# The earliest best cluster by halving sums on GpSimd, in place of a second maximum on VectorE

## The chip, the cores and the metric

The kernel runs on one core of one Trainium2 chip. The metric is the device time of one execution in microseconds (us). Engines are named as in the profile: PE is TensorE (PEld its weight loads), DVE is VectorE, ACT is ScalarE, POOL is GpSimd, SP is SyncE, which here issues all transfers.

## The reference

Clustered attention, then two feed-forward blocks, all in float32. Two batches, 8 heads, 768 positions, head dimension 64, 16 clusters. Each query and each key is assigned to the cluster whose centroid it is most similar to; a query attends only to keys of its own cluster. Where two clusters are equally good, `argmax` gives the earlier one.

```python
q_assign = np.argmax(np.einsum('bhsd,hcd->bhsc', q_n, c_n), axis=-1)
k_assign = np.argmax(np.einsum('bhsd,hcd->bhsc', k_n, c_n), axis=-1)
mask = q_assign[:, :, :, None] == k_assign[:, :, None, :]
scores = np.where(mask, 0.125 * np.matmul(q, k.transpose(0, 1, 3, 2)), -1e9)
attn = softmax(scores) @ v                     # 2 x 8 x 768 x 64
x = attn as 1536 x 512
x = ((x @ w1) * (x @ w2)) @ w3 @ w_out         # 1024 wide inside
h = x @ w_in                                   # 2048 wide
out = (np.maximum(h, 0) + alpha * np.minimum(h, 0)) @ w_out2
```

## The kernel before

Each engine has its own program, written out by hand; semaphores join them. Every product is made from high and low halves of its operands, in three matmuls or, for the scores, four.

**Stages.** A setup (about 70 us) loads and splits weights, multiplies the two middle matrices into one, and prepares the first heads. Attention follows, to about 295 us, then the feed-forward blocks.

**Attention.** The 16 heads are taken in 4 turns of 4 heads; a head has 6 tiles of 128 queries, so a turn has 24 tiles, and `step(it, c, last)` is one tile's step on each engine: each engine has its own version, and the order inside it is the engine's queue. PE in step c makes the scores of tile c (`score`), transposes probabilities of group c - 4 (`turn_probabilities`, line 689, in two halves b = 0, 1), does what `prepared` lists, and multiplies group c - 5 with v (`weigh`). DVE in step c takes the row maximum of tile c (`maximum`, line 1200), then the low halves `pl` of group c - 4 (`probabilities_lo`, line 1206, a pair of instructions), then what `prepared` lists, then in one step of six the reciprocal of the row sums (`inverse`, line 1212). ACT makes exponentials, the high halves `ph`, and copies of finished output (line 982). PE's transposition of group g, half b, waits for `pl` of group g - 1, half b. POOL handles clusters (`picks`), the split of v (lines 489, 493), the addition of epsilon to the row sums (line 531), and adds, scales and splits the finished output of two heads (lines 541, 545, 551, 558).

**Clusters.** Once in 12 steps, for two heads together. PE makes the similarities (steps 2 and 3 of 12), DVE transposes them so that each of 128 partitions holds 24 positions with 32 values (`ct`, line 1181). Then, before the change:

1. POOL adds the high and low contributions: 24 x 16 values `c16` (line 509, step 4).
2. DVE takes their maximum over 16, `cmx` (line 1190, step 4).
3. POOL subtracts it, compares with zero, and multiplies by the weights 16, 15, ..., 1 (lines 511, 513, 514). A best cluster keeps its weight, the others are 0.
4. DVE takes a second maximum (line 1193, step 6): the weight of the earliest best one.
5. POOL adjusts it (518), subtracts it (519) and turns the result into the rows `oh` by maximum and multiplication (521): query rows and key rows get values such that their product in the scores pushes pairs of different clusters far down.
6. DVE transposes `oh` back (line 1196, step 8), and SP sends eight small transfers of it into the operands of the two heads (`masks`, line 327). PE waits for them at the first tile of each head.

Between some POOL instructions stands a small one of 1 x 2 elements into `spare` (lines 512, 517, 520). POOL waits for each of its own instructions by a semaphore before it starts the next of the chain (`ordered_step`).

The places of this work in a turn are given by `prepared`, which all engines use: "pick1" in step 4 of 12, "pick2" in step 6, "pick3" in step 8.

Of the kernel before, what the change touches and what calls it, by code (L numbers as in the profile page):

```python
# [34 lines left out]
FAR = 2.0 ** 60  # L35
SCALE = D ** -0.5
HB = 4
# [10 lines left out]
FILLS = 6  # L48
# [6 lines left out]
def prepared(it, c, last):  # L55

    j, m = c // 12 * 2, c % 12
    plan = {0: [("turned", j + 3, 0)], 1: [("turned", j + 3, 1)], 2: [("cluster", j + 2, 0)], 3: [("cluster", j + 2, 1)],
            4: [("pick1", j + 2, 0)], 6: [("pick2", j + 2, 0)], 8: [("pick3", j + 2, 0)],
            10: [("turned", j + 4, 0)], 11: [("turned", j + 4, 1)]}.get(m, [])  # L60
    there = HB if last else 2 * HB if isinstance(it, int) and it == TURNS - 2 else 3 * HB
    return [(kind, head, half) for kind, head, half in plan if head < there]
# [7 lines left out]
def finished(c):  # L70

    j, u = divmod(c - T6 - LX, T6)
    return (j, u) if 0 <= j < HB else (None, None)
# [8 lines left out]
def inverted_now(c, last, lag):  # L82

    j, t = divmod(c - T6, T6)
    return j if t == lag and j >= 0 and (not last or j < HB) else None


def build(nc, q, k, v, cen, w1, w2, w3, wo, w_in, w_out, alpha, out):
    ctx = ExitStack()
    with ctx:  # L90
        def sem(name):
            return ctx.enter_context(nc.semaphore(name))

        def sb(name, shape, dt=F32, where=ctx):
            return where.enter_context(nc.sbuf_tensor(name, shape, dt))
# [17 lines left out]
        zero = al[:, NJ:NJ + T6]  # L113
# [116 lines left out]

        block = ctx.enter_context(nc.Block())

        POOL_SETUP = 16 + HB
        CEN_DVE = 6
        CLUS = 9
        W12_EARLY = len(W12_STEPS)
        W34_EARLY = NF + 1
        X_FREE, FOLD_FREE = 2, 1
# [209 lines left out]
        def _(pool):  # L448
            count = [0]

            def ordered(ins):
                count[0] += 1
                ins.then_inc(setup_pool, 1)
                pool.wait_ge(setup_pool, count[0])
# [3 lines left out]
                                            base=0, pattern=[[-1, P]], channel_multiplier=1))  # L458
# [2 lines left out]
            ordered(nc.gpsimd.memset(scl[0:D, :], SCALE))  # L461
            ordered(nc.gpsimd.memset(zero[:, :], 0.0))
            ordered(nc.gpsimd.memset(epsilon[:, :], 1e-9))
            ordered(nc.gpsimd.iota(wts[:, :], pattern=[[-1, NCL]], base=NCL, channel_multiplier=0,
                                   allow_small_or_imprecise_dtypes=True))
            for j in range(1, HB):
                ordered(nc.gpsimd.memset(cwin[j][:, :].bitcast(F32), 0.0))
            ordered(nc.gpsimd.memset(oh[:, :, :, :], 0.0))
            ordered(nc.gpsimd.memset(far[:, 0:1], 0.0))
            ordered(nc.gpsimd.memset(far[:, 1:3], 1.0))  # L470
            for e in range(2):
                ordered(nc.gpsimd.memset(far[64 * e:64 * e + 32, 0:1], -1.0))
                ordered(nc.gpsimd.memset(far[64 * e:64 * e + 32, 1:2], FAR))
                ordered(nc.gpsimd.memset(far[64 * e:64 * e + 32, 2:3], 0.0))
            assert count[0] == POOL_SETUP

            def window(it, j):
# [16 lines left out]
                                        v12[e][:, :, x_rows(j)].bitcast(F32), ALU.subtract).then_inc(v_done, 1)  # L494
                pool.wait_ge(v_done, n + 1)

            def picks(it, j, part):

                pair = 2 * it + j // 2
                ct3 = ct[:, :].rearrange("p (b c) -> p b c", c=32)  # L500
                over = lambda x: x[:, :].unsqueeze(2).to_broadcast([P, 24, NCL])
                weights = wts[:, :].unsqueeze(1).to_broadcast([P, 24, NCL])
                def ordered_step(k, ins):
                    ins.then_inc(clus_step, 1)
                    pool.wait_ge(clus_step, CLUS * pair + k)

                if part == 1:
                    pool.wait_ge(prep_free, FILLS * (pair + 1))
                    ordered_step(1, nc.gpsimd.tensor_tensor(c16[:, :, :], ct3[:, :, 0:NCL], ct3[:, :, NCL:2 * NCL], ALU.add))
                    pool.wait_ge(clus_step, CLUS * pair + 2)  # L510
                    ordered_step(3, nc.gpsimd.tensor_tensor(c16[:, :, :], c16[:, :, :], over(cmx), ALU.subtract))
                    nc.gpsimd.tensor_tensor(spare[0:1, 0:2], zero[0:1, 0:2], zero[0:1, 0:2], ALU.add)
                    ordered_step(4, nc.gpsimd.tensor_scalar(c16[:, :, :], c16[:, :, :], 0.0, None, ALU.is_ge))
                    ordered_step(5, nc.gpsimd.tensor_tensor(c16[:, :, :], c16[:, :, :], weights, ALU.mult))
                else:
                    pool.wait_ge(clus_step, CLUS * pair + 6)
                    nc.gpsimd.tensor_tensor(spare[0:1, 0:2], zero[0:1, 0:2], zero[0:1, 0:2], ALU.add)
                    ordered_step(7, nc.gpsimd.tensor_scalar(cmx[:, :], cmx[:, :], far[:, 2:3], None, ALU.subtract))
                    ordered_step(8, nc.gpsimd.tensor_tensor(c16[:, :, :], c16[:, :, :], over(cmx), ALU.subtract))
                    nc.gpsimd.tensor_tensor(spare[0:1, 0:2], zero[0:1, 0:2], zero[0:1, 0:2], ALU.add)  # L520
# [42 lines left out]
            def step(it, c, last):  # L563
                j, t = divmod(c, T6)
                out_head, u = finished(c)
                for kind, h, _ in prepared(it, c, last):
                    if kind in ("pick1", "pick2"):
                        picks(it, h, int(kind[4]))
# [26 lines left out]
            picks(0, 0, 1)  # L595
            picks(0, 0, 2)
            split_v(0, 0)
            for c in range(LEAD):
                step(0, c, False)
# [522 lines left out]
        def _(dve):  # L1122
# [61 lines left out]
            def picks(it, j, part):  # L1184


                pair = 2 * it + j // 2
                if part == 1:
                    dve.wait_ge(clus_step, CLUS * pair + 1)
                    nc.vector.tensor_reduce(cmx[:, :], c16[:, :, :], AX.X, ALU.max).then_inc(clus_step, 1)  # L1190
                elif part == 2:
                    dve.wait_ge(clus_step, CLUS * pair + 5)
                    nc.vector.tensor_reduce(cmx[:, :], c16[:, :, :], AX.X, ALU.max).then_inc(clus_step, 1)
                else:
                    dve.wait_ge(clus_step, CLUS * pair + CLUS)
                    nc.vector.transpose(ct[:, 0:HS], oh[:, 0, :, :].rearrange("p b c -> p (b c)")).then_inc(onehot_done, 1)
# [52 lines left out]
            picks(0, 0, 2)  # L1249
            picks(0, 0, 3)  # L1250
            w3_lo_part(6, 0)
            for half in range(2):
# [108 lines left out]
```

## Time and profile before

| what | value |
|---|---|
| median of 3 runs | 747.94 us (747.90 to 747.99) |
| the profiled execution | 747.64 us, its span 745.8 us |
| PE busy | 739.0 us (99%), granted clock 0.999 |
| DVE, ACT, POOL busy | 411.8, 311.6, 179.5 us |
| SP | issues all transfers; the 16 DMA engines moved 54 MB |
| chain that ended last | PE 97%, DVE 1%, DMA 1% |

The span runs from the first instruction to the last; the time has another 1.8 us around it. A start time is counted from the span's start. Durations overlap a little: an instruction can start before the one ahead of it on its engine has fully ended, so that start to start is shorter than the sum of durations. Lines of the profile with "x2" or "x6" hold that many instructions of one kind in a row.

### The profile page before, as it was taken

Reading aid. Unit: us, or ns where it says so; the run is one execution under the profiler, and the core shown is the slowest. Engines: PE = TensorE matmul, PEld = TensorE weight load, DVE = VectorE, ACT = ScalarE, POOL = GpSimd, SP = SyncE. Lnnn points to the kernel's source line nnn. Section 1 sums busy time; section 2 is a strip of 40 time slices with the busy share of each in tenths; the row PEclk is TensorE's granted clock in tenths of the full one; section 3 lists DMA queues with packets and bytes.
Section 4 is the critical chain, followed back from the end, with each engine's and each line's share of the span. In section 5 each row is a group of like instructions: output and inputs, shape, how many; then the busy total and the mean of one; then the engine's idle time right before and its main releaser. Section 6 shows DMA issues by size and latency. Waiting matters only on the chain.

```text
span 745.8 us, 10690 instructions
## 1 busy us (share of the span) xinstructions
PE 739.0 (99%) x3792; PEld 641.6 (86%) x3792; DVE 411.8 (55%) x632; ACT 311.6 (42%) x623; POOL 179.5 (24%) x211
## 2 busy tenths in 40 slices
PE   8999999999999999999999999999999999999998
PEld 6888999999999998888888888888888888888886
DVE  4435999999999984721311432575434333343432
ACT  5235988988988884311211422432012111121111
POOL 2141566866865893500000000000000000000000
PEclk9999999999999999999999999999999999999999
DMA  9636366566566233300000022140001000010001
GB/s 293 195 94 144 78 152 155 124 146 154 127 146 153 65 84 92 98 29 1 1 0 1 20 93 85 57 130 11 1 0 57 1 0 1 1 56 1 1 0 57
DMA packets 65371, 54.17 MB, mean 73 GB/s; under 512 B 32032, under 2 KB 54576, under 8 KB 65328
## 3 DMA queue, kind: packets, MB, share of 16 engines
q1 hardware_dynamic: 65328, 53.59, 27.9%
q8 instruction: 28, 0.46, 0.3%
q14 instruction: 15, 0.12, 0.1%
HBM read 31.50 MB, written 3.19 MB: 47 GB/s over the span
## 4 chain that ended last, share of the span: by engine, by line
PE 97%; DVE 1%; DMA 1%; ACT 1%; issue 0%; SPq 0%; DVEq 0%; ACTq 0%
PE slot L625 63%; PE acc L625 24%; PE slot L689 9%; PE acc L638 1%; PE slot L737 1%; DMA early<-in_moe_w_out 1%; DVE xl L1163 0%; DVE xl L1145 0%; ACT xh L938 0%; ACT xh L945 0%; DVE abx L1283 0%; DVE ab L1279 0%; ACT abx L1055 0%; ACT asb L1041 0%; ACT ost L1108 0%
## 5 line engine op out<-in xcount | busy, mean ns | idle before, releaser
L625 PE MATMUL slot<-xh,w 128*128 128x512 f32 x768 | 248.0, 389 | 0.0
L625 PEld LDWEIGHTS slot<-xh,w 128*128 128x128 f32 x768 | 144.1, 188 | 29.8
L625 PE MATMUL slot<-xl,w 128*128 128x512 f32 x384 | 149.4, 389 | 0.0
L1101 ACT CAST gh<-gf 128x512 fp32r<-128x512 f32 x48 | 29.9, 623 | 203.2 <-PE acc L625 186.0
L1206 DVE TENSOR_TENSOR pl<-slot,ph 128x384 fp32r<-128x384 f32 x192 | 97.6, 549 | 8.5 <-ACT ph L973 8.2
L1200 DVE TENSOR_REDUCE nm<-slot 128x1 f32<-128x768 f32 x96 | 91.4, 952 | 15.4 <-PE slot L625 13.8
L973 ACT CAST ph<-slot 128x384 fp32r<-128x384 f32 x192 | 83.5, 489 | 34.3 <-PE slot L689 33.8
L965 ACT ACTIVATE pf<-slot,nm 128x768 f32<-128x768 f32 x96 | 88.4, 921 | 4.6 <-DVE nm L1200 4.5
L625 PEld LDWEIGHTS slot<-xl,w 128*128 128x128 f32 x384 | 72.1, 188 | 15.0
L625 PE MATMUL slot<-k,q 80*128 80x384 f32 (+1 forms) x384 | 82.9, 337 | 0.0
L1329 DVE TENSOR_TENSOR gl<-gf,gh 128x512 fp32r<-128x512 f32 x48 | 33.2, 692 | 89.9 <-ACT gh L1101 89.9
L689 PE MATMUL slot<-ident,pf 128*128 128x128 f32 x576 | 79.4, 273 | 0.2
L689 PEld LDWEIGHTS slot<-ident,pf 128*128 128x128 f32 x576 | 68.5, 140 | 5.4 <-DVE pl L1206 1.4
L625 PE MATMUL acc<-ph,v 128*128 128x384 f32 x192 | 71.7, 373 | 0.0
L625 PEld LDWEIGHTS slot<-k,q 80*128 80x128 f32 (+1 forms) x384 | 68.6, 188 | 0.3
L1279 DVE TENSOR_TENSOR ab<-slot,asb 128x512 f32<-128x512 f32 x24 | 16.5, 690 | 90.2 <-ACT asb L1041 90.2
L1322 DVE TENSOR_SCALAR neg<-slot,al 128x512 f32<-128x512 f32 x48 | 36.0, 750 | 52.1 <-PE slot L625 52.1
L625 PE MATMUL acc<-pl,v 128*128 128x384 f32 x192 | 64.7, 337 | 0.0
L625 PE MATMUL slot<-w,gh 128*128 128x512 f32 x192 | 59.1, 389 | 0.0
L625 PE MATMUL acc<-w,gh 128*128 128x512 f32 x192 | 59.1, 389 | 0.0
L1041 ACT COPY asb<-slot 128x512 f32<-128x512 f32 x24 | 14.1, 588 | 103.1 <-PE slot L625 103.1
L625 PEld LDWEIGHTS acc<-w,gh 128*128 128x128 f32 x192 | 36.0, 188 | 7.4
(121 smaller groups left out, 1012.0 us busy)
## 6 DMA issues: line engine op xcount, KB each, us to landing
stage<-in_moe_w SPq DMA_DIRECT2D x16, 256.0 KB, 3.5
stage<-in_moe_w_in SPq DMA_DIRECT2D x16, 256.0 KB, 2.7
stage<-in_moe_w_out SPq DMA_DIRECT2D x16, 256.0 KB, 3.0
stage<-in_moe_w SPq DMA_DIRECT2D x6, 512.0 KB, 4.2
qk<-in_q SPq DMA_DIRECT2D x16, 192.0 KB, 3.9
qk<-in_k SPq DMA_DIRECT2D x16, 192.0 KB, 3.9
vn<-in_v SPq DMA_DIRECT2D x16, 192.0 KB, 3.8
q<-k SPq DMA_DIRECT2D x16, 192.0 KB, 3.8
```

The lines of the kernel that those rows point to most:

```text
L625: return nc.tensor.matmul(o, a, b, start=start, stop=stop)
L638: last = nc.tensor.transpose(o[:, t * P:(t + 1) * P], qk[j % 2][:, 3 * half + t, :, :].rearrange("p a d -> p (a d)"), ident[:, :])
L689: last = nc.tensor.transpose(turned_p[:, b, i * P:(i + 1) * P], p[:, key_tile * P:(key_tile + 1) * P], ident[:, :])
L965: nc.scalar.activation(pf[c % NPF][:, :, :], wide(scores[c % 2]), ACT.Exp, bias=nm[:, c % 4:c % 4 + 1], accum_out=sm[j % 2][:, t:t + 1]).t ...
L973: copy(ph[g % NPH][:, b, :], turned_p[:, b, 0:HS]).then_inc(ph_done, 1)
L1041: copy(asb[f % 2][:, :], bank[2 * (f % 2)]).then_inc(asb_done, 1)
L1101: copy(gh[j % 2][:, :], gf[j % 2][:, :]).then_inc(gh_done, 1)
L1200: nc.vector.tensor_reduce(nm[:, c % 4:c % 4 + 1], wide(scores[c % 2]), AX.XY, ALU.max, negate=True).then_inc(max_done, 1)
L1206: tt_(pl[g % NPH][:, b, :], turned_p[:, b, 0:HS], f32(ph[g % NPH][:, b, :]), ALU.subtract).then_inc(pl_done, 1)
L1279: tt_(ab[f % 2][:, :], bank[2 * (f % 2) + 1], asb[f % 2][:, :], ALU.mult).then_inc(ab_done, 1)
L1322: ts(neg[:, :], h, 0.0, al[:, j:j + 1], ALU.min, ALU.mult).then_inc(neg_done, 1)
L1329: tt_(gl[j % 2][:, :], gf[j % 2][:, :], f32(gh[j % 2][:, :]), ALU.subtract).then_inc(gl_done, 1)
```

## The change

The weights 16 to 1 become powers of two, FAR times 2^16 down to FAR times 2 (FAR is 2^60). After the comparison and the multiplication, POOL adds up the 16 values of a position in four halvings (16 to 8, 4, 2, 1, written into unused columns of `oh`). In a sum of different powers of two the largest is more than half of the sum, so half of the sum separates the earliest best cluster from all others: POOL halves the sum, subtracts it, and makes `oh` by maximum and minimum. DVE's second maximum is gone, and with it step "pick2"; POOL does the whole of `picks` in step 4. DVE's transposition stays in step 8. Sixteen memsets make the weights in the setup where one `iota` did, and the constants `far` lose a column.

```diff
-            4: [("pick1", j + 2, 0)], 6: [("pick2", j + 2, 0)], 8: [("pick3", j + 2, 0)],
+            4: [("pick1", j + 2, 0)], 8: [("pick3", j + 2, 0)],
...
-            ordered(nc.gpsimd.iota(wts[:, :], pattern=[[-1, NCL]], base=NCL, channel_multiplier=0,
-                                   allow_small_or_imprecise_dtypes=True))
+            for c in range(NCL):
+                ordered(nc.gpsimd.memset(wts[:, c:c + 1], FAR * 2.0 ** (NCL - c)))
...
-            def picks(it, j, part):
+            def picks(it, j):
...
+                spot = oh[:, 1, :, :].rearrange("p b c -> p (b c)")
+                sums = [spot[:, 24 * n:48 * n].rearrange("p (b c) -> p b c", c=n) for n in (8, 4, 2, 1)]
+                total = sums[3].rearrange("p b c -> p (b c)")
...
                 ordered_step(5, nc.gpsimd.tensor_tensor(c16[:, :, :], c16[:, :, :], weights, ALU.mult))
-                else:
-                    pool.wait_ge(clus_step, CLUS * pair + 6)
-                    nc.gpsimd.tensor_tensor(spare[0:1, 0:2], zero[0:1, 0:2], zero[0:1, 0:2], ALU.add)
-                    ordered_step(7, nc.gpsimd.tensor_scalar(cmx[:, :], cmx[:, :], far[:, 2:3], None, ALU.subtract))
-                    ordered_step(8, nc.gpsimd.tensor_tensor(c16[:, :, :], c16[:, :, :], over(cmx), ALU.subtract))
-                    nc.gpsimd.tensor_tensor(spare[0:1, 0:2], zero[0:1, 0:2], zero[0:1, 0:2], ALU.add)
-                    ordered_step(9, nc.gpsimd.tensor_scalar(
-                        oh[:, 0, :, :].rearrange("p b (a c) -> p a b c", a=2),
-                        c16[:, :, :].rearrange("p (a b) c -> p a b c", a=2), far[:, 0:1], far[:, 1:2], ALU.max, ALU.mult))
+                k = 5
+                for n, (x, y) in enumerate(zip([c16] + sums, sums)):
+                    w = y.shape[2]
+                    ordered_step(k + n + 1, nc.gpsimd.tensor_tensor(y[:, :, :], x[:, :, 0:w], x[:, :, w:2 * w], ALU.add))
+                nc.gpsimd.tensor_tensor(spare[0:1, 0:2], zero[0:1, 0:2], zero[0:1, 0:2], ALU.add)
+                ordered_step(k + 5, nc.gpsimd.tensor_scalar(total, total, 0.5, None, ALU.mult))
+                ordered_step(k + 6, nc.gpsimd.tensor_tensor(c16[:, :, :], c16[:, :, :], over(total), ALU.subtract))
+                nc.gpsimd.tensor_tensor(spare[0:1, 0:2], zero[0:1, 0:2], zero[0:1, 0:2], ALU.add)
+                ordered_step(k + 7, nc.gpsimd.tensor_scalar(
+                    oh[:, 0, :, :].rearrange("p b (a c) -> p a b c", a=2),
+                    c16[:, :, :].rearrange("p (a b) c -> p a b c", a=2), far[:, 0:1], far[:, 1:2], ALU.max, ALU.min))
...
-                elif part == 2:
-                    dve.wait_ge(clus_step, CLUS * pair + 5)
-                    nc.vector.tensor_reduce(cmx[:, :], c16[:, :, :], AX.X, ALU.max).then_inc(clus_step, 1)
```

## Rows read from the trace of the kernel before

**Rows 1.** Busy times by window: stretch, PE, PEld, DVE, ACT, POOL, clock, DMA.

```profile
120.00:160.00 40.00, 40.00 (x271) 38.99 (x270) 38.50 (x68) 33.93 (x80) 24.98 (x33) 1.00 0.67 152
```

**Rows 2.** Timeline of DVE: start us, duration us, engine, line, operation.

```profile
129.37 0.96 DVE L1200 TENSOR_REDUCE nm<-slot 128x1 f32<-128x768 f32 x1
...
131.18 0.54 DVE L1193 TENSOR_REDUCE cmx<-c 128x24 f32<-128x384 f32 x1
131.64 0.95 DVE L1200 TENSOR_REDUCE nm<-slot 128x1 f32<-128x768 f32 x1
...
135.33 0.57 DVE L1196 STREAM_TRANSPOSE ct<-oh 128x384 f32<-128x384 f32 x1
...
136.66 1.00 DVE L1206 TENSOR_TENSOR pl<-slot,ph 128x384 fp32r<-128x384 f32 x2
...
138.66 1.01 DVE L1206 TENSOR_TENSOR pl<-slot,ph 128x384 fp32r<-128x384 f32 x2
```

**Rows 3.** Timeline of PE and its weight loads, same pair of heads.

```profile
131.80 0.42 PE L625 MATMUL acc<-ph,v 128*128 128x384 f32 x1
...
134.03 0.19 PEld L625 LDWEIGHTS acc<-ph,v 128*128 128x128 f32 x1 [0.16 <-ACT xf L982]
...
138.24 0.49 PE L638 MATMUL acc<-ident,qk 128*128 128x128 f32 x3
...
140.62 0.49 PE L638 MATMUL acc<-ident,qk 128*128 128x128 f32 x3
...
141.64 0.86 PE L625 MATMUL slot<-k,q 128*128 128x384 f32 x4
```

**Rows 4.** Timeline around 71 us, where PE waited for DVE.

```profile
70.60 1.02 DVE L1206 TENSOR_TENSOR pl<-slot,ph 128x384 fp32r<-128x384 f32 x2
...
71.68 0.31 PEld L689 LDWEIGHTS slot<-ident,pf 128*128 128x128 f32 x3 [0.15 <-DVE pl L1206]
...
71.98 0.42 PE L625 MATMUL acc<-ph,v 128*128 128x384 f32 x1
```

**Rows 5.** Line 509 by itself: ns min/median/max, first and last start.

```profile
L509 POOL TENSOR_TENSOR c<-ct x8: 1008/1014/1022, 35.1 to 236.2; 128x384 f32<-128x384 f32 x8
```

**Rows 6.** Timeline of POOL, the pair of rows 2 and 3.

```profile
129.86 1.02 POOL L514 TENSOR_TENSOR c<-c,wts 128x384 f32<-128x384 f32 x1
131.80 0.18 POOL L517 TENSOR_TENSOR spare<-al 1x2 f32<-1x2 f32 x1 [0.92 <-DVE cmx L1193]
...
133.48 1.64 POOL L521 TENSOR_SCALAR oh<-c,far 128x384 f32<-128x384 f32 x1
```

**Rows 7.** Groups of POOL: shapes, count, busy us, mean ns, idle before.

```profile
L545 POOL TENSOR_TENSOR xf<-xf,rep 128x768 f32<-128x768 f32 x8 | 18.8, 2350 | 0.6
...
L513 POOL TENSOR_SCALAR c<-c 128x384 f32<-128x384 f32 x8 | 9.4, 1172 | 0.0
...
L558 POOL TENSOR_TENSOR xl<-xf,xh 128x768 f32 x4 | 7.4, 1838 | 0.7 <-POOL xh L551 0.7
```

**Rows 8.** Timelines of POOL and DVE in the setup.

```profile
42.39 0.18 POOL L517 TENSOR_TENSOR spare<-al 1x2 f32<-1x2 f32 x1 [2.09 <-DVE cmx L1193]
...
44.08 1.64 POOL L521 TENSOR_SCALAR oh<-c,far 128x384 f32<-128x384 f32 x1
...
45.75 0.58 DVE L1196 STREAM_TRANSPOSE ct<-oh 128x384 f32<-128x384 f32 x1 [3.51 <-POOL oh L521]
```

**Rows 9.** Timelines of POOL and DVE at the first place in attention.

```profile
76.31 0.18 POOL L517 TENSOR_TENSOR spare<-al 1x2 f32<-1x2 f32 x1 [0.73 <-DVE cmx L1193]
...
77.99 1.64 POOL L521 TENSOR_SCALAR oh<-c,far 128x384 f32<-128x384 f32 x1
...
79.81 0.57 DVE L1196 STREAM_TRANSPOSE ct<-oh 128x384 f32<-128x384 f32 x1
```

**Rows 10.** DMA issues: size, us to landing; and the fourth mask transfer on SP.

```profile
q<-ct SPq DMA_DIRECT2D x4, 24.0 KB, 1.9
...
137.84 0.59 SPq L327 DMA_DIRECT2D k<-ct  x1
```

More of the change, by code:

```diff
@@ L231, in build @@
         block = ctx.enter_context(nc.Block())
-        POOL_SETUP = 16 + HB
+        POOL_SETUP = 13 + NCL + HB
         CEN_DVE = 6
-        CLUS = 9
+        CLUS = 12
         W12_EARLY = len(W12_STEPS)
@@ L469, in _ @@
             ordered(nc.gpsimd.memset(far[:, 0:1], 0.0))
-            ordered(nc.gpsimd.memset(far[:, 1:3], 1.0))
+            ordered(nc.gpsimd.memset(far[:, 1:2], FAR))
             for e in range(2):
                 ordered(nc.gpsimd.memset(far[64 * e:64 * e + 32, 0:1], -1.0))
-                ordered(nc.gpsimd.memset(far[64 * e:64 * e + 32, 1:2], FAR))
-                ordered(nc.gpsimd.memset(far[64 * e:64 * e + 32, 2:3], 0.0))
+                ordered(nc.gpsimd.memset(far[64 * e:64 * e + 32, 1:2], 0.0))
             assert count[0] == POOL_SETUP
@@ L495, in split_v @@
                 pool.wait_ge(v_done, n + 1)
-            def picks(it, j, part):
+            def picks(it, j):
                 pair = 2 * it + j // 2
                 ct3 = ct[:, :].rearrange("p (b c) -> p b c", c=32)
-                over = lambda x: x[:, :].unsqueeze(2).to_broadcast([P, 24, NCL])
+                over = lambda x: x.unsqueeze(2).to_broadcast([P, 24, NCL])
                 weights = wts[:, :].unsqueeze(1).to_broadcast([P, 24, NCL])
+                spot = oh[:, 1, :, :].rearrange("p b c -> p (b c)")
+                sums = [spot[:, 24 * n:48 * n].rearrange("p (b c) -> p b c", c=n) for n in (8, 4, 2, 1)]
+                total = sums[3].rearrange("p b c -> p (b c)")
                 def ordered_step(k, ins):
@@ L505, in ordered_step @@
                     pool.wait_ge(clus_step, CLUS * pair + k)
[L507 to L511, printed above, removed]
-                    nc.gpsimd.tensor_tensor(spare[0:1, 0:2], zero[0:1, 0:2], zero[0:1, 0:2], ALU.add)
-                    ordered_step(4, nc.gpsimd.tensor_scalar(c16[:, :, :], c16[:, :, :], 0.0, None, ALU.is_ge))
-                    ordered_step(5, nc.gpsimd.tensor_tensor(c16[:, :, :], c16[:, :, :], weights, ALU.mult))
-                else:
-                    pool.wait_ge(clus_step, CLUS * pair + 6)
-                    nc.gpsimd.tensor_tensor(spare[0:1, 0:2], zero[0:1, 0:2], zero[0:1, 0:2], ALU.add)
-                    ordered_step(7, nc.gpsimd.tensor_scalar(cmx[:, :], cmx[:, :], far[:, 2:3], None, ALU.subtract))
-                    ordered_step(8, nc.gpsimd.tensor_tensor(c16[:, :, :], c16[:, :, :], over(cmx), ALU.subtract))
-                    nc.gpsimd.tensor_tensor(spare[0:1, 0:2], zero[0:1, 0:2], zero[0:1, 0:2], ALU.add)
-                    ordered_step(9, nc.gpsimd.tensor_scalar(
-                        oh[:, 0, :, :].rearrange("p b (a c) -> p a b c", a=2),
-                        c16[:, :, :].rearrange("p (a b) c -> p a b c", a=2), far[:, 0:1], far[:, 1:2], ALU.max, ALU.mult))
@@ new lines, in picks @@
+                pool.wait_ge(prep_free, FILLS * (pair + 1))
+                ordered_step(1, nc.gpsimd.tensor_tensor(c16[:, :, :], ct3[:, :, 0:NCL], ct3[:, :, NCL:2 * NCL], ALU.add))
+                pool.wait_ge(clus_step, CLUS * pair + 2)
+                ordered_step(3, nc.gpsimd.tensor_tensor(c16[:, :, :], c16[:, :, :], over(cmx[:, :]), ALU.subtract))
+                nc.gpsimd.tensor_tensor(spare[0:1, 0:2], zero[0:1, 0:2], zero[0:1, 0:2], ALU.add)
+                ordered_step(4, nc.gpsimd.tensor_scalar(c16[:, :, :], c16[:, :, :], 0.0, None, ALU.is_ge))
@@ new lines, in picks @@
+                ordered_step(5, nc.gpsimd.tensor_tensor(c16[:, :, :], c16[:, :, :], weights, ALU.mult))
+                k = 5
[4 more added lines that the diff above has]
+                ordered_step(k + 5, nc.gpsimd.tensor_scalar(total, total, 0.5, None, ALU.mult))
@@ L525, in add_epsilon @@
+                ordered_step(k + 6, nc.gpsimd.tensor_tensor(c16[:, :, :], c16[:, :, :], over(total), ALU.subtract))
+                nc.gpsimd.tensor_tensor(spare[0:1, 0:2], zero[0:1, 0:2], zero[0:1, 0:2], ALU.add)
+                ordered_step(k + 7, nc.gpsimd.tensor_scalar(
+                    oh[:, 0, :, :].rearrange("p b (a c) -> p a b c", a=2),
+                    c16[:, :, :].rearrange("p (a b) c -> p a b c", a=2), far[:, 0:1], far[:, 1:2], ALU.max, ALU.min))
             def add_epsilon(it, j):
@@ L566, in step @@
                 for kind, h, _ in prepared(it, c, last):
-                    if kind in ("pick1", "pick2"):
-                        picks(it, h, int(kind[4]))
+                    if kind == "pick1":
+                        picks(it, h)
                 if t == 0 and c > 0 and (not last or j < HB):
@@ L594, in _ @@
             pool.wait_ge(folded, FOLD_FREE)
-            picks(0, 0, 1)
-            picks(0, 0, 2)
+            picks(0, 0)
             split_v(0, 0)
@@ L1248, in _ @@
             w3_lo_part(5, 1)
-            picks(0, 0, 2)
             picks(0, 0, 3)
```

## The prediction

> **What bounds the kernel now.** I read the page's slices first, for the stage in which the edit lies, then the busy times of a stretch of it: in 40 us of attention TensorE (PE) is busy for 40.00 and VectorE (DVE) for 38.50 [rows 1]. Both look full, so the shares don't say which sets the pace. The timelines do. In the tile with the second cluster maximum DVE is 2.27 us from row maximum to row maximum; the cluster maximum holds 0.46 of it (start to start), so an unburdened tile needs 1.81 on DVE [rows 2]. PE's groups around the same tile stand 2.23 apart, of which 0.16 is a wait for a ScalarE copy: 2.07 of work [rows 3]. So PE sets the pace, with DVE close behind, and the reader should see this: DVE may be late by a small amount and no more.
>
> How much is read where the next step needs it. PE's second transposition of tile group 6 waits for the second `pl` of group 5. Where PE really waited for such a `pl`, the pair on DVE ended at 71.62, and PE's next kind of work started at 71.98, 0.36 us behind the pair's end [rows 4]. In the pair of heads that I work out, the `pl` pair of group 5 ends at 137.66 (136.66 plus 1.00), so PE could go on at 138.02; it does at 138.24 [rows 2, 3]. The slack is **0.22 us**.
>
> **The change part by part.** Once in 12 tiles both engines work on the clusters of two heads: the eight places begin on GpSimd from 35.1 to 236.2 us [rows 5]; the first lies in the setup, seven in attention.
>
> Removed on DVE: one maximum of 0.54 us, 0.46 start to start [rows 2], eight times, 3.7 us. It gives PE nothing directly, as PE sets the pace; at most the row maximum behind it starts 0.1 to 0.2 sooner, ScalarE's exponential and copy follow, and PE's 0.16 of waiting shrinks, by about 0.12.
>
> GpSimd's chain. Until the multiplication by weights ends at 130.88 it is as before. Then it waited 0.92 us for DVE's maximum, and from 131.80 the small filler, a `tensor_scalar` of 24, the subtraction and the last operation ran on to 135.12 [rows 6]. These four kinds remain (0.5 in place of a pointer, minimum in place of multiplication; taken at no difference). In place of the wait stand four additions of 192, 96, 48 and 24 elements. Two-input operations of 384 and of 768 elements take 1014 and 1838 ns, which makes 2.14 ns an element and 0.19 us fixed; the filler of 2 elements, at 0.18, lies on that line [rows 5 to 7]. So the four cost 0.60, 0.40, 0.29 and 0.24, together 1.53 us, and with 0.08 between ordered operations (as from DVE's maximum, done at 131.72, to GpSimd's start at 131.80 [rows 2, 6]) 1.85. With 0.08 ahead of the first, 1.93 takes the place of 0.92: the chain ends **1.01 us later**, at 136.13.
>
> Lower bound: each halving at the two-element filler's 0.18 us, 1.05 us with gaps; then the chain ends 0.21 later. Upper bound: the nearest dear row is the last operation, which writes 24 runs with gaps and takes 1.64, 0.47 more than the `tensor_scalar` on the same 384 elements [rows 6, 7]; 0.47 on each halving would be 1.9 us more a time. I take the line, because the addition that reads both inputs in runs of 16 with gaps is the very one of 1014 ns [rows 5]: it lies on one line with operations on whole rows. Between them lies the multiplication whose second input is read with a step of 24 bytes, 2350 against 1838 ns [rows 7]: 0.67 ns an element, 0.24 us for the 360 elements of four halvings.
>
> A rule of the Trainium skill bears on that last row: the GPSIMD Engine Reference, section 7 (Performance pitfalls for Q7 kernels), has half as much again an element for reads with an inner step over 8 bytes. The row with 24 bytes agrees in kind; by the rule the halvings (step 4 bytes, and 8 in the last) pay nothing and the sum stays as it is, by the row's surcharge on all it would be 1.7 us more. Section 4.1 of the same page (Engine selection) sends a reduction along the free dimension to VectorE, which speaks against this change: here 0.54 us there against 1.53 on GpSimd by the line above.
>
> What waits for the chain. DVE's transposition of the one-hot rows is in DVE's fixed order behind the `pl` pair of step 8; it started at 135.33, with no idle time before it, GpSimd having finished at 135.12 [rows 2, 6]. Now it can start at 136.16 (0.03 for the release, as 45.72 to 45.75 in the setup, where DVE did wait for it [rows 8]): DVE stands still for **0.83 us**. That DVE had one operation less two tiles earlier doesn't help; it arrives at this place by PE's pace. Queued behind the transposition are row maximum 9, the `pl` pair of group 5, and the reciprocal of the row sums; ScalarE waits for the maximum and PE for the pair. The pair ends 0.83 later, PE uses up 0.22 of slack, and PE stands **0.61 us**. The 0.12 that PE might have won before is swallowed too, since this wait hangs on GpSimd's chain and not on PE.
>
> The reciprocal needs GpSimd's addition of epsilon, which stands behind the chain in GpSimd's order and comes 1.01 later, so DVE may be 1.01 late from there on. Does that cost PE again? PE's next such place has 0.59 us of slack (the next `pl` pair ends at 139.67, PE went on at 140.62, less 0.36 [rows 2, 3]), and DVE's lateness beyond PE's own is 0.4: no. PE works longer in the two later tiles with cluster scores, and DVE catches up there. Nothing is given back to PE.
>
> First place in attention: the wait removed was 0.73, so the chain ends 1.20 later, 80.86 with the release against 79.81: 1.05 of standing, less 0.22: loss **0.83** [rows 9]. I count the other six at 0.61: 3.66. In the setup DVE already waited 3.51 us for GpSimd, and the removed wait of 2.09 was longer than the 1.93 put in [rows 8]: 0.16 sooner, and what DVE does next waits for ScalarE: nothing. The 13 more memsets there, at no more than the filler's 0.18 and 0.08, take 3.4 us between the start and 35.1, where GpSimd waits for DVE's cluster scores anyway [rows 5].
>
> SyncE's queue: the mask transfers go out 0.83 later; the fourth went out at 137.84 and such a transfer lands 1.9 us behind its issue [rows 10], 139.7, then 140.6; PE's first matmul that needs it starts at 141.64 [rows 3], 142.25 then. Slack 1.6, no cost. What GpSimd does behind the chain (splitting v, normalising) is 1.01 late as well, 0.4 against PE; PE waits for none of it in the trace, and I count nothing.
>
> Sum: 0.83 + 3.66 = 4.5 us. The profiled execution took 747.64 (span 745.8 and 1.8 around it), so 752.1; the median of the runs shown is 0.3 higher, **752.4 us**, 0.6% slower. A change under 0.2%, 1.5 us, can't be told from none here.
>
> **The rivals.** (a) As forecast, but dearer halvings. With the 24-byte row's surcharge 754.1; with half the upper bound, 0.95 more a place, 759. For it: short runs, never seen below 16. Against: the row with runs of 16. (b) PE absorbs it: no change. The halvings would have to cost so little, or DVE's slack be so much more than 0.22, that under 0.2 a place is left: 748 to 749.4. For it: the filler's 0.18, and the next place shows 0.59 of slack. Against: the line through three rows. (c) Faster: DVE and not PE is the bound in attention, so that each removed maximum is worth its 0.46: 7 x 0.46 = 3.2, 744.7; with only PE's 0.12 back, 747.1. It decides the sign if the chain ends before 135.3, which needs the four halvings in under 1.05 us with their gaps, the lower bound. For it: DVE's 38.50 of 40. Against: PE's 2.07 of work in the very tile in which DVE carries the maximum. (d) Contention: 12 us more of GpSimd slows DVE. The `pl` pairs take 1.00 to 1.02 us at every place shown, under whatever GpSimd does [rows 2, 4]; I give it nothing of its own.
>
> **How the numbers follow.** Forecast 0.66, dearer 0.16, absorbed 0.11, faster 0.07. Slower by over 0.2%: 0.82; within: 0.11; faster: 0.07. The range leaves out the last two cases and the far end of the first rival: 749.6 to 756.0. It takes in the 24-byte row above and, below, half of the price per element, 0.39 us less at seven places (749.7).
>
> **What would show it.** DVE idle before the one-hot transposition, 0.8 us six times and 1.05 once, released by GpSimd's last operation, where now only the setup has such a wait. PE's transpositions waiting for `pl` in seven more places, two waits each, 0.6 in sum. GpSimd 12 us busier, DVE 4.3 less. The pairs' first GpSimd operations 28.3 us apart in place of 27.7. The stages behind attention equal to 0.1 us. Wrong would be: halvings of 0.2 us each; DVE's transposition back to back with the `pl` before it; or PE unmoved at a DVE that stands 0.8.

## The result and the profile after

| | before | after |
|---|---|---|
| median of 6 runs each | 747.91 us (747.67 to 747.99) | 751.82 us (751.67 to 752.33) |
| profiled execution, its span | 747.64, 745.8 us | 751.73, 749.9 us |
| DVE, POOL busy | 411.8, 179.5 us | 408.0, 191.7 us |

The ratio is 1.0055, with an interval of 1.0044 to 1.0065: slower by 3.9 us. The forecast was 752.4. One disturbed execution of before_first_max_sooner, of 818.5 us at a mean clock of 0.851, is left out of the bounds given for it below.

GpSimd's groups in the kernel after, different shapes apart (line, tiles, shapes, count, then busy us, mean ns of one, idle before), give each new operation its price:

```profile
L526 POOL TENSOR_SCALAR oh<-c,far 128x384 f32<-128x384 f32 x8 | 13.1, 1640 | 0.0
...
L521 POOL TENSOR_TENSOR oh<-c 128x192 f32<-128x192 f32 x8 | 4.8, 594 | 0.6
...
L521 POOL TENSOR_TENSOR oh<-oh 128x96 f32<-128x96 f32 x8 | 3.1, 388 | 0.6
L521 POOL TENSOR_TENSOR oh<-oh 128x48 f32<-128x48 f32 x8 | 2.1, 266 | 0.6
L523 POOL TENSOR_SCALAR oh<-oh 128x24 f32<-128x24 f32 x8 | 2.1, 265 | 0.0
L521 POOL TENSOR_TENSOR oh<-oh 128x24 f32<-128x24 f32 x8 | 1.8, 225 | 0.6
```

The four halvings take 1.47 us together. Each also has 0.08 us of idle time before it (0.6 over eight): every operation waits for the one before.

The chain that answers to [rows 6], timeline of GpSimd (start, duration):

```profile
131.04 1.02 POOL L517 TENSOR_TENSOR c<-c,wts 128x384 f32<-128x384 f32 x1
132.14 0.59 POOL L521 TENSOR_TENSOR oh<-c 128x192 f32<-128x192 f32 x1
132.82 1.03 POOL L521 TENSOR_TENSOR oh<-oh 128x96 f32<-128x96 f32 x3
...
134.09 0.27 POOL L523 TENSOR_SCALAR oh<-oh 128x24 f32<-128x24 f32 x1
...
135.54 1.64 POOL L526 TENSOR_SCALAR oh<-c,far 128x384 f32<-128x384 f32 x1
...
139.50 0.20 POOL L536 TENSOR_TENSOR rec<-sm,epsilon 128x6 f32<-128x6 f32 x1 [0.24 <-POOL v L492]
```

DVE in the same pair of heads, as in [rows 2]:

```profile
135.55 1.01 DVE L1207 TENSOR_TENSOR pl<-slot,ph 128x384 fp32r<-128x384 f32 x2
137.21 0.58 DVE L1197 STREAM_TRANSPOSE ct<-oh 128x384 f32<-128x384 f32 x1 [0.65 <-POOL oh L526]
137.71 0.92 DVE L1201 TENSOR_REDUCE nm<-slot 128x1 f32<-128x768 f32 x1
138.56 1.01 DVE L1207 TENSOR_TENSOR pl<-slot,ph 128x384 fp32r<-128x384 f32 x2
139.73 0.19 DVE L1213 RECIPROCAL rec<-rec 128x6 f32<-128x6 f32 x1 [0.17 <-POOL rec L536]
```

The transposition stood back to back with the `pl` pair before it in [rows 2]; now 0.65 us of idle time lie between them, ended by GpSimd's last operation at 137.18 (135.54 plus 1.64). And the weight loads of PE, to be held against [rows 3]:

```profile
139.15 0.31 PEld L693 LDWEIGHTS slot<-ident,pf 128*128 128x128 f32 x3 [0.63 <-DVE pl L1207]
139.62 0.31 PEld L693 LDWEIGHTS slot<-ident,pf 128*128 128x128 f32 x3 [0.15 <-DVE pl L1207]
```

That is the whole path: GpSimd's chain ends late, DVE's transposition waits for it, the row maximum and the `pl` pair behind it come late, and PE waits for both halves of `pl`, one after the other.

The waits summed over the run (total us, times, longest):

```profile
DVE ct L1197 <- POOL oh L526: 8.5, 8, 3.7
...
PEld slot L693 <- DVE pl L1207: 4.6, 14, 0.6
...
PE slot L693 <- DVE pl L1207: 2.3, 7, 0.5
```

The first two lines of before were 3.5 us in one wait, the setup's, and 1.4 us in six. The third, with one wait of PE's matmuls at each of the seven places, was not there. (The weight loads' line names `pl` at four of the seven, twice each; at the other three they wait 0.59 to 0.76 us and no releaser is named.) The eight waits of DVE are 3.7 in the setup, 0.82 in the first place of attention and 0.64 to 0.67 in the other six.

To see the cost to the kernel and not to one engine, I take the starts of the first GpSimd operation of each pair. Before they were 66.92, 97.06, 124.79, 152.51, 180.31, 208.24 and 236.18 us; now they are 66.77, 97.68, 125.98, 154.27, 182.57, 211.04 and 239.49. The first distance grew from 30.14 to 30.91, the others by 0.57, 0.57, 0.50, 0.54 and 0.51 us. Together 3.46 us, less the 0.15 by which the first start is sooner: 3.31.

The seventh place has no such start behind it. There DVE's row maxima of both kernels, held against each other, show the shift: 3.31 us at the last one ahead of the transposition (244.82 us before), 4.07 from 253.49 on, 4.12 at the last one in attention (276.72), 4.10 for DVE's last operations (734.18). So the seventh place cost 0.76. PE waits twice there:

```profile
252.72 0.71 PEld L693 LDWEIGHTS slot<-ident,pf 128*128 128x128 f32 x6 [0.61 <-issue]
...
256.56 0.65 PEld L629 LDWEIGHTS slot<-k,q 128*128 128x128 f32 x4 [0.36 <-issue]
```

Behind the first wait PE's products start at 253.42 for 249.59, 0.52 more than the 3.31. The second wait, for the scores two tiles later, brings the rest; the profile names nothing that released it.

### The profile page after: what moved, and what is told of

The parts are those of the page before. It is cut to its first block, busy times and chain, and to the rows that moved or that the text cites. A ratio compares the mean times of both kernels' runs of the same rounds, so it can differ in the third digit from the quotient of the medians.

```text
span 749.9 us, 10731 instructions
## 1 busy us (share of the span) xinstructions
PE 740.8 (99%) x3792; PEld 641.0 (85%) x3792; DVE 408.0 (54%) x624; ACT 312.3 (42%) x623; POOL 191.7 (26%) x256
## 4 chain that ended last, share of the span: by engine, by line
PE 77%; POOL 13%; issue 5%; DVE 3%; ACT 1%; POOLq 1%; DVEq 0%; ACTq 0%
PE slot L629 56%; PE acc L629 17%; PE slot L693 3%; POOL oh L526 2%; POOL oh L521 1%; POOL c L516 1%; POOL c L517 1%; POOL xf L550 1%; POOL v L492 1%; POOL c L514 1%; POOL c L524 1%; POOL xl L563 1%; POOL xf L546 1%; DVE nm L1201 1%; PE acc L642 1%
## 5 line engine op out<-in xcount | busy, mean ns | idle before, releaser
L1201 DVE TENSOR_REDUCE nm<-slot 128x1 f32<-128x768 f32 x96 | 91.2, 950 | 17.9 <-PE slot L629 15.8
```

Source lines behind the costliest of these rows:

```text
L1201: nc.vector.tensor_reduce(nm[:, c % 4:c % 4 + 1], wide(scores[c % 2]), AX.XY, ALU.max, negate=True).then_inc(max_done, 1)
```

## The experiments

The theory at this point: the loss is DVE's idle time before the transposition, handed to PE less a small slack; removing the maximum gives nothing back. The rivals: DVE's removed maximum was worth something, hidden under a dearer chain; or the loss lies elsewhere, in GpSimd's contention, in the reciprocal or in the masks. All medians below are in us; each ratio is to the kernel before, measured beside it at 747.7 to 748.0. The diffs are cut down to what matters: where steps of the chain are added or taken, their numbering and the count `CLUS` change too.

### Length of the chain and the removed maximum, one at a time

**one_halving**, made from the kernel after:

```diff
-                for n, (x, y) in enumerate(zip([c16] + sums, sums)):
-                    w = y.shape[2]
-                    ordered_step(k + n + 1, nc.gpsimd.tensor_tensor(y[:, :, :], x[:, :, 0:w], x[:, :, w:2 * w], ALU.add))
+                y = sums[3]
+                ordered_step(k + 1, nc.gpsimd.tensor_tensor(y[:, :, :], c16[:, :, 0:1], c16[:, :, 1:2], ALU.add))
```

> The changed kernel with only the last of the four halvings, one addition of 24 elements on two of the 16 columns (so the chosen clusters are wrong in this run; all other work is done). GpSimd's chain is 1.49 us shorter a place than in the changed kernel (592 + 388 + 266 ns and three gaps of 0.08), and VectorE has the one maximum less. Forecast's theory (VectorE stands for the chain, TensorE sets the pace otherwise): no idle time before the one-hot transposition except in the setup, the 3.9 us come back, and up to 0.16 at seven places on top where TensorE waited for ScalarE's copy: 746.9 to 747.9 us. Rival that VectorE is the bound in attention: each removed maximum is worth 0.46, so 744.7. Rival that something other than the chain's length costs (more instructions, the missing place in the order): it stays near 751.8.

747.52, ratio 0.9995 (0.9986 to 1.0004). The chosen clusters are wrong in this kernel, its other work is the same. Now the chain is shorter than before's, and only the setup's wait is left:

```profile
DVE ct L1196 <- POOL oh L525: 2.2, 1, 2.2
```

This is the cleanest bound on the benefit: the second maximum is gone, nothing waits in its place, and the kernel is 0.35 us faster by medians, with an interval that spans zero (1.0 us faster to 0.3 slower). Seven removed maxima at 0.46 would have been 3.2 us. DVE wasn't the bound.

**five_halvings**, the first addition done twice:

```diff
+                    if n == 0:
+                        ordered_step(k + 1, nc.gpsimd.tensor_tensor(y[:, :, :], x[:, :, 0:w], x[:, :, w:2 * w], ALU.add))
```

> The changed kernel with the first halving done twice, the same result: the chain is 0.67 us longer a place (0.59 and a gap). Theory: every 0.67 reaches TensorE, seven times, 4.7 more than the changed kernel: 756.5 us, and the places 28.9 to 29.0 us apart. Rival that the loss is not the chain's length: 751.8. Rival that VectorE's lateness then also bites at the place behind it (0.59 of slack): over 757.

756.35, ratio 1.0114 (1.0098 to 1.0129). DVE and PE in the same pair:

```profile
139.37 0.58 DVE L1199 STREAM_TRANSPOSE ct<-oh 128x384 f32<-128x384 f32 x1 [1.33 <-POOL oh L528]
```

```profile
141.31 0.31 PEld L695 LDWEIGHTS slot<-ident,pf 128*128 128x128 f32 x3 [1.28 <-DVE pl L1209]
```

One addition more is 0.67 us with its gap (0.59 plus 0.08). DVE's idle time grew by 0.68, PE's wait by 0.65, and the time by 4.53 us, 0.65 for each of seven places. Once the slack is used up, what is added to GpSimd's chain is added to the kernel nearly in full (0.65 of 0.67), seven times.

**unused_maximum** gives DVE a maximum of the same shape back in step 6, of a constant, into a tile that nobody reads:

```diff
-            4: [("pick1", j + 2, 0)], 8: [("pick3", j + 2, 0)],
+            4: [("pick1", j + 2, 0)], 6: [("pick2", j + 2, 0)], 8: [("pick3", j + 2, 0)],
...
+                elif part == 2:
+                    nc.vector.tensor_reduce(unused[:, :], ident[:, 0:NCL].unsqueeze(1).to_broadcast([P, 24, NCL]), AX.X, ALU.max)
```

> The changed kernel, with a maximum over 24 times 16 elements put back on VectorE in step 6, of a constant tile and with no wait on either side; its result is unused. Theory: VectorE stands 0.65 us two tiles later anyway, so the 0.46 fit into that: 751.8 us, as the changed kernel, within 0.3. Rival that the removed maximum brought back part of the loss (VectorE the bound): up to 3.2 more, 755.0.

751.94, ratio 1.0056 (1.0043 to 1.0070): the kernel after, within 0.12 us. DVE's stand in the same pair:

```profile
137.27 0.58 DVE L1200 STREAM_TRANSPOSE ct<-oh 128x384 f32<-128x384 f32 x1 [0.61 <-POOL oh L527]
```

The time is as expected, the reason given is not: of the 0.46 only 0.04 went into the stand (0.61 for 0.65). The rest went into the idle time before DVE's row maxima, in which it waits for PE's scores: 14.0 us over the run in place of 15.8. With DVE as the bound there would be no such time to fill, and the stand would have shrunk by the whole 0.46. So a maximum more or less in this place is worth nothing that can be measured, from this side too.

**before_longer_chain** leaves the second maximum in the kernel before and puts two additions of 144 elements behind it on GpSimd:

```diff
+                    for n in range(2):
+                        ordered_step(7 + n, nc.gpsimd.tensor_tensor(
+                            spot[:, 0:144], spot[:, 144:288], spot[:, 144:288], ALU.add))
```

> The kernel before, both maxima on VectorE, with two additions of 144 elements into unused columns put into GpSimd's chain behind the second maximum: by the line 0.50 and 0.08 each, 1.16 us longer a place; the result is the same. Theory: VectorE stands about 1.0 us before the transposition, TensorE loses about 0.77, seven times 5.4, so 753.3 us; up to 0.5 more if TensorE feels the 1.16 in the setup. That would be the change's loss without its removal. Rival that TensorE has more slack than 0.22: under 750.

752.63, ratio 1.0064 (1.0050 to 1.0078). DVE's wait at the transposition:

```profile
DVE ct L1200 <- POOL oh L525: 10.1, 8, 4.5
```

```profile
L519 POOL TENSOR_TENSOR oh<-oh 128x144 f32<-128x144 f32 x16 | 6.8, 428 | 9.0 <-DVE cmx L1197 8.3
```

The loss of the change, and a little more, appears in a kernel that never lost its maximum. The additions were 428 ns, not the 0.50 us of the expectation, so the chain grew by 1.02 and not 1.16; the time was 0.7 under the 753.3 expected.

### The same work, with the chain started sooner

DVE's first cluster maximum (line 1194) is moved ahead of the `pl` pair of step 4, so that GpSimd can subtract about 1 us sooner. No work is added or taken. **after_first_max_sooner** and, from the kernel before, **before_first_max_sooner**:

```diff
                     maximum(it, c)
+                for kind, j, _ in prepared(it, c, last):
+                    if kind == "pick1":
+                        picks(it, j, 1)
                 if there(c - LT):
                     probabilities_lo(it, c - LT)
...
-                    else:
+                    elif kind != "pick1":
                         picks(it, j, int(kind[4]))
```

> The changed kernel with VectorE's cluster maximum of step 4 put ahead of the pl pair of that step in place of behind it. GpSimd's chain starts 0.9 us sooner and ends some 0.3 before VectorE comes to the transposition: no wait there. In return the pl pair of step 4 is 0.46 late; its end plus 0.36 then lies 0.12 behind the place where TensorE goes on now. Theory: 747.5 (the run with one halving) plus 7 times 0.12, 748.3 us; the loss is a matter of when the chain starts, not of GpSimd's work. Rival that GpSimd's extra 12 us cost in themselves: it stays above 750. Rival that the pl pair has no slack in step 4 either: 747.5 plus 7 times 0.46, 750.7.

> The control: the same move in the kernel before, where no one waits for the chain. Theory: only the cost of the later pl pair remains, 7 times 0.12, 748.7 us. If this lies above 750, the pl pair of step 4 has no slack.

747.97, ratio 1.0004 (0.9995 to 1.0012), and 748.39 (748.10 to 748.75), ratio 1.0009 (1.0000 to 1.0018). In the first, timeline of DVE:

```profile
134.74 1.01 DVE L1207 TENSOR_TENSOR pl<-slot,ph 128x384 fp32r<-128x384 f32 x2
135.67 0.57 DVE L1197 STREAM_TRANSPOSE ct<-oh 128x384 f32<-128x384 f32 x1
136.16 0.92 DVE L1201 TENSOR_REDUCE nm<-slot 128x1 f32<-128x768 f32 x1
```

and its weight loads, four steps earlier:

```profile
127.29 0.31 PEld L693 LDWEIGHTS slot<-ident,pf 128*128 128x128 f32 x3 [0.22 <-DVE pl L1207]
127.75 0.31 PEld L693 LDWEIGHTS slot<-ident,pf 128*128 128x128 f32 x3 [0.15 <-DVE pl L1207]
```

The transposition is back to back again and the whole loss is gone, although GpSimd still does its 12 us more. That rules out contention as the cause, and with it the amount of GpSimd's work: what counts is when its chain ends. The small price of the order is where expected: the `pl` pair of step 4 now stands behind the maximum, and PE waits for it there; the places are 27.75 to 27.93 us apart, against 27.72 to 27.94 before. The version is the kernel before's equal, no faster.

### The transposition moved later: three hooks behind one chain

If the transposition's place is what turns the chain into lost time, a later place should free it. **after_transpose_step9** changes one number of the plan that all queues share:

```diff
-            4: [("pick1", j + 2, 0)], 8: [("pick3", j + 2, 0)],
+            4: [("pick1", j + 2, 0)], 9: [("pick3", j + 2, 0)],
```

> The changed kernel with VectorE's one-hot transposition, and the mask transfers behind it on SyncE, in step 9 in place of 8. VectorE no longer stands: the chain has ended by then. But the fourth mask transfer leaves at about 140.1 on the clock of the kernel before and lands 1.9 later, at 142.0, where TensorE's first matmul of the next head wants to start at 141.6. Theory: the wait for GpSimd goes and a wait for the masks of some 0.4 to 0.5 takes its place, seven times: 750.5 to 751. Rival that the transfers are not needed so soon or land sooner: 747.5. Rival that the loss was never VectorE's standing: 751.8.

780.27 (776.33 to 783.22), ratio 1.0423 (1.0397 to 1.0449). The expectation was wrong by 29 us. DVE's wait did go, but PE now waits for the masks:

```profile
117.76 1.14 PEld L629 LDWEIGHTS slot<-k,q 128*128 128x128 f32 x4 [2.99 <-DMA k<-ct]
...
150.43 0.65 PEld L629 LDWEIGHTS slot<-k,q 128*128 128x128 f32 x4 [2.91 <-DMA k<-ct]
```

Why so late? The transposition was done at 143.49, but the first mask transfer went out at 146.62. SyncE's queue and GpSimd's, same stretch:

```profile
145.99 0.52 SPq L336 DMA_DIRECT2D xo<-xf  x1
146.62 0.60 SPq L327 DMA_DIRECT2D q<-ct  x1
...
148.53 0.59 SPq L327 DMA_DIRECT2D k<-ct  x1
```

```profile
143.79 0.20 POOL L536 TENSOR_TENSOR rec<-sm,epsilon 128x6 f32<-128x6 f32 x1 [0.24 <-POOL v L492]
144.06 1.85 POOL L546 TENSOR_TENSOR xf<-xf,xo 128x768 f32<-128x768 f32 x1
```

In step 9 the masks stand in SyncE's queue behind `xo<-xf`, which may overwrite `xo` only when GpSimd's addition (line 546) has read it: done at 145.91, issued at 145.99. That addition stands behind the same chain on GpSimd. The masks waited for a transfer that waited for the engine that is late. The fourth mask went out at 148.53 and PE went on at 150.43, 1.9 behind, as in [rows 10].

A stand of 3 us had a second cost. Windows of the same execution (busy of PE, PEld, DVE, ACT, POOL, then the granted clock):

```profile
117.00:119.00 2.00, 1.24 (x4) 1.24 (x5) 0.00 (x0) 0.00 (x0) 1.83 (x2) 0.64 0.16 37
119.00:121.00 2.00, 2.00 (x12) 1.90 (x10) 1.36 (x2) 0.76 (x2) 1.68 (x3) 0.51 0.30 36
121.00:123.00 2.00, 2.00 (x15) 1.97 (x14) 1.66 (x4) 1.67 (x5) 0.53 (x2) 1.00 0.74 191
```

Behind the wait of 2.99 us PE came back at 0.51 of its clock, the 1.2 GHz level, and was at 1.00 again from 121. Four matmuls took 1.65 us there, against 0.88 in the same form at 137.97 in the kernel after. The low level doesn't last equally long each time: behind the stand that ended at 183.22 the rows up to 189 are at 0.50. I don't know why. The mean clock from 97.5 to 163.0 is 0.95, from 163.0 to 265.2 it is 0.90; 5% of a pair of 32.8 us is 1.6 us, 10% of 34 is 3.4. Wait and clock together make distances of 32.7 to 34.2 in place of 28.3.

**transpose_step9_masks_kept** moves DVE's transposition alone and leaves the masks at step 8 in SyncE's queue (DVE's loop goes through `prepared(it, c - 1, last)` for "pick3"):

> As the run before, VectorE's one-hot transposition in step 9, but the mask transfers keep their place of step 8 in SyncE's order, ahead of the transfer of finished output (xo) that waits for GpSimd's addition behind the chain. Theory: the 32 us of the run before were that place in the queue (masks behind a transfer that waits for GpSimd's later work), so they vanish; left is the masks' own lateness, the fourth landing at 142.0 against 141.5, seven times 0.4 to 0.5: 750.5 to 751. Rival that the transposition's place on VectorE costs in itself: it stays above 770. Rival that the masks have more slack than I count: 747.5.

752.32, ratio 1.0057 (1.0043 to 1.0070). The 28 us are gone with the masks' place in the queue, so that cause is shown. But the median is 1.3 us above the expectation's 751, and nothing is won against the kernel after. DVE's next wait in its place:

```profile
139.91 0.19 DVE L1213 RECIPROCAL rec<-rec 128x6 f32<-128x6 f32 x1 [0.50 <-POOL rec L536]
```

The reciprocal needs GpSimd's addition of epsilon (line 536), behind the chain too. In this order it stands in step 9 behind the transposition, DVE waits for it, and the following `pl` is late: PE waits 0.34 and 0.15 at 141.48 and 141.94, and 0.21 more for its operands.

**transpose_behind_row_max** puts the transposition behind the row maximum of step 9 and ahead of the `pl` pair:

```diff
                     maximum(it, c)
+                for kind, j, _ in prepared(it, c - 1, last):
+                    if kind == "pick3":
+                        picks(it, j, 3)
                 if there(c - LT):
                     probabilities_lo(it, c - LT)
...
-                    else:
+                    elif kind != "pick3":
                         picks(it, j, int(kind[4]))
```

> The changed kernel with the one-hot transposition on VectorE between row maximum 9 and the pl pair of group 5, masks at their place on SyncE. GpSimd's chain has ended by then, so no wait for it; the pl pair has the transposition's 0.49 ahead of it as in the kernel before, but the row maximum can't start before its scores, so the pair comes some 0.35 later than before. Theory: 0.35 less the slack of 0.22, 0.1 to 0.25 a place: 748.3 to 749.3. Rival that the slack is nearer to 0.6: 747.5. Rival that what costs is GpSimd's lateness for the reciprocal and the output work: 751 or more.

750.91, ratio 1.0040 (1.0027 to 1.0054): above the expected 749.3 and next to the rival's 751. Both had a part. The transposition itself no longer waits. PE waits 0.22 and 0.15 for the `pl` pair at 138.43 and 138.89, as the expectation had it; but at 139.35 the reciprocal waits 0.51 on DVE too, and PE waits 0.21 for its operands at 141.91.

So I took the reciprocal a step later as well, in three kernels: **transpose_step9_reciprocal_later**, **transpose_behind_row_max_reciprocal_later**, and as a control **after_reciprocal_later**, where the transposition stays:

```diff
-                j = inverted_now(c, last, 3)
+                j = inverted_now(c, last, 4)
```

> The transposition in step 9 with the masks at their place, and VectorE's reciprocal of the row sums one step later, in step 10. In the run without the latter VectorE stood 0.50 us in front of the reciprocal, for GpSimd's addition of epsilon, which lies behind the whole chain, and TensorE lost 0.6 a place there. Theory that this second wait is the whole of that run's loss: 747.5. With the masks just too late as well (fourth landing 0.2 to 0.4 behind the scores' start): 748.5 to 750. Rival that something else holds TensorE there: 752.3 as before.

750.92, ratio 1.0041 (1.0027 to 1.0054). The reciprocal's wait is gone, 1.4 us are back, and the masks are the next hook:

```profile
142.76 0.65 PEld L629 LDWEIGHTS slot<-k,q 128*128 128x128 f32 x4 [0.44 <-DMA k<-ct]
```

The fourth mask went out at 140.86 and PE went on 1.9 later. The transposition started at 138.35, because its place behind the `pl` pair of step 9 is as late as that.

> The transposition behind row maximum 9, and the reciprocal in step 10. Two waits of TensorE were seen in the run without the latter: 0.22 and 0.15 at the pl of group 5, and a second at the operands one step later, behind VectorE's 0.51 in front of the reciprocal. Theory: the second goes, the first stays, 0.1 to 0.2 a place: 748.3 to 749.2. Rival that the reciprocal is no part of it: 750.9.

749.49, ratio 1.0021 (1.0012 to 1.0030). Only the two waits of 0.24 and 0.16 for the `pl` pair are left, at 138.22 and 138.69, since the pair now stands behind the transposition. The reciprocal's part was 1.4 us (749.49 for 750.91), the pair's is the 1.5 that are left. Of the 3.9 us lost 2.3 are back.

> The changed kernel with the reciprocal one step later and nothing else. There VectorE's wait for GpSimd in front of the reciprocal is 0.16 us only, behind the wait at the transposition. Theory of the prediction (the next place has slack for it): 751.8, the same within 0.3. Rival that this second wait has a part in the 3.9 us: 750.7, 0.16 sooner at seven places.

752.03, ratio 1.0052 (1.0038 to 1.0066), DVE's wait at the transposition 0.66 and PE's 0.61, as in the kernel after. The reciprocal has no part in the change's loss; it costs only where the transposition's wait has been taken away in front of it.

## Why the prediction was right, point by point

- **PE sets the pace, the removed maximum gives nothing.** Right, and shown from both sides: 0.35 us by medians with the wait away (one_halving; the interval reaches 1.0), 0.12 the other way with the maximum back (unused_maximum). DVE's 38.50 of 40 us in [rows 1] was no sign of the bound. Rival (c), 744.7 to 747.1, falls by one_halving: at 747.52 even without the longer chain the maxima bring nothing that can be told from none.
- **The halvings.** The line gave 0.60, 0.40, 0.29 and 0.24; measured 594, 388, 266 and 225 ns, 1.47 in place of 1.53 us. No surcharge for runs of 8, 4, 2 and 1 elements, so rival (a) falls. The Trainium skill (GPSIMD Engine Reference, section 7, Performance pitfalls for Q7 kernels) puts the surcharge on an inner step of over 8 bytes only; the last halving, with a step of 8 bytes, agrees at 225 ns. The small `tensor_scalar` was taken at no difference; it takes 265 ns for 333. Both together make the chain 0.14 shorter than worked out: counted from its first addition it ends at 11.20 us (137.18 less 125.98), against 10.33 before (135.12 less 124.79), 0.87 later and not 1.01.
- **DVE's stand.** The 0.83 of the prediction is how much later the transposition starts. Measured in the same way it is 0.69: 11.23 us after the first addition (137.21 less 125.98) against 10.54 (135.33 less 124.79). The 0.14 between them are the chain's. The profile's idle time of 0.65 counts from the end of the `pl` pair, which the transposition overlapped by 0.08 when it didn't wait; DVE arrives no later than before, its pair starts 9.57 us after the first addition for 9.60. At the first place it is 0.89 (13.78 for 12.89) where 1.05 was predicted.
- **The slack.** This term was mis-sized the other way. I took 0.36 us from the pair's end to PE's next work, read where that work was a product with v [rows 4]. In the place that counts the next work is the transposition of operands, and after a real wait it starts 0.43 behind the pair's end (138.56 plus 1.01, then 140.00, PE's row for line 642). At the seventh place, where a product follows at once, it is 0.35 again (252.06 plus 1.01, then 253.42). So the slack was 0.15 and not 0.22. The pair came 0.71 later in its place (12.58 against 11.87), PE 0.57 (14.02 against 13.45).
- **The sum.** Five places 0.50 to 0.57 for 0.61, the first 0.77 for 0.83, the seventh 0.76 for 0.61; in all 4.1 us of the profiled time (751.73 less 747.64) for 4.5. It came out so near with some luck: the stand was 0.14 too long, the slack 0.07 too large, and the seventh place's second wait was not in it. That the late end of the chain makes the loss is shown by five_halvings, before_longer_chain and after_first_max_sooner. Rival (b), absorbed, needed under 0.2 us a place to be left; it was 0.50 or more. Rival (d), contention, falls by after_first_max_sooner.
- **No further cost.** Right at six places: the reciprocal waits 0.17 where DVE was said to be up to 1.01 late, and PE doesn't wait for it (after_reciprocal_later). Wrong at the seventh, by about 0.24 us, where PE waits again two tiles later. The masks: right in the kernel after, which shows no wait of PE for them. But the slack of 1.6 us that I gave them holds for the transposition's place, not for any: with the transposition a step later it was overdrawn by 0.44.
- **The setup.** Nothing was predicted to arrive from there, and nothing does. The transposition comes 10.33 us after the chain's start in place of 10.64, 0.31 sooner (0.16 predicted, 0.14 more by the shorter chain). But from that start to the next pair's it is 31.76 us for 31.81. The 0.15 by which this pair is sooner (66.77 for 66.92) are mostly there already at the chain's start (35.01 for 35.11), which lies between 34.84 and 35.38 in the kernels measured.
- **What would show it.** Distances of 28.3 (28.3), PE's waits for `pl` in seven more places, stages behind attention equal (the shift is 4.12 us at their start and 4.10 at their end): all there. GpSimd is 12.2 us busier for 12, but the 12 were the halvings alone, which are 11.8; the sixteen memsets add 1.6, and the `tensor_scalar` and what else got shorter or went away take 1.2 off. DVE is 3.8 less busy for 4.3: eight times 0.54 counted the overlap with the next operation too, eight times 0.46 are 3.7. What stays open is what released PE's second wait at the seventh place.

## What to carry to other kernels

An operation is worth what its place in the queues makes of it: before moving work to an engine with time to spare, list what on the fuller engines waits for the chain, what is queued behind that wait, and the slack to the first thing that the pace-setting engine needs; beyond the slack every microsecond counts in full, here seven times. When one such hook is removed the next stands close behind (here the transposition, the reciprocal, the masks), and a place in a plan that DMA queues share moves the transfers as well, past others that may wait for the same late engine. Read the slack at the very place, with the same kind of work behind it: 0.36 from another place and 0.43 in the right one made a difference of a third of it.

## What the runs showed of the hardware

- A PE that stood 2.99 us came back at the 1.2 GHz level, a granted clock of 0.51, and was at 1.00 again 3 us later (121 us); behind another such stand the low level lasted some 6 us (183 to 189 us). By the mean clock of each pair I estimate that this added 1.6 to 3.4 us a pair to the wait. Waits of up to 1.3 us, in five_halvings, left the clock of the whole execution at 1.0.
- The addition of 144 elements whose two inputs are the same tile took 428 ns; the line through 192 and 96 elements with two different inputs (594 and 388) gives 491 at 144. Whether the shared input is the reason wasn't tried. In the kernel before a subtraction of 384 elements whose second input is one value repeated 16 times (line 511) took 842 ns, and the addition of two different inputs (line 509) 1014.
- The `tensor_scalar` of 24 elements took 265 ns with a constant; in the kernel before, with a pointer to a value per partition, it took 333. The last operation cost the same with minimum as with multiplication (1640 ns, start to end 1.64 in [rows 6] too).
